# Retention, mixture of experts and MLP on one core: unstacked outputs, paced loads, shifted weight rounding

## The reference

```python
scores = scale * q @ k.T                  # batch 2, heads 8, sequence 576, head size 64
ret = scores * Dmat                       # gamma_h ** (i - j) for i >= j, else 0
x = ret @ v                               # as 1152 tokens x 512
for e in range(4):                        # mixture of experts, F = 1024
    out += p[:, e] * (relu(x @ w1[e]) @ w2[e])
h = out @ w_in                            # MLP, 2048 wide
y = (h * tanh(softplus(h))) @ w_out
```

## Time and profile before

| | us |
|---|---|
| median of three runs (lowest, highest) | 621.39 (620.98, 622.14) |
| profiled execution: its own time | 619.39 |
| profiled execution: span | 617.3 |
| PE busy | 604.9 (98% of the span) |
| PE weight loads busy | 546.4 (89%) |
| DVE, ACT, POOL busy | 265.1, 234.8, 278.5 (43%, 38%, 45%) |
| mean granted TensorE clock, share of full | 0.997 |
| DMA, mean | 82 GB/s |

### The profile page before, as it was taken

How to read it: one execution, slowest core, us unless ns; L and a number is a source line. 1 busy time by engine, 2 the same in 40 slices (tenths; PEclk the granted TensorE clock), 3 DMA queues, 4 the chain that set the end, 5 groups by cost and what they waited for, 6 DMA issues and landing times.

```text
span 617.3 us, 9709 instructions
## 1 busy us (share of the span) xinstructions
PE 604.9 (98%) x3952; PEld 546.4 (89%) x3952; DVE 265.1 (43%) x365; ACT 234.8 (38%) x434; POOL 278.5 (45%) x230
## 2 busy tenths in 40 slices
PE   7799999999999999999999999999999999999997
PEld 5788999999899999999999999989989999989996
DVE  5477654323254433154434154535545432334334
ACT  2466244322233321323332223435455454334431
POOL 2668645534435535335554435532446543443300
PEclk9899999999999999999999999999999999999999
DMA  9963222322112332012331112321112232201002
GB/s 345 340 225 103 72 66 65 109 72 64 35 34 69 107 100 69 34 35 69 102 102 54 50 35 69 103 68 52 52 35 65 67 101 75 69 0 52 2 0 103
DMA packets 24923, 50.47 MB, mean 82 GB/s; under 512 B 2864, under 2 KB 2992, under 8 KB 24880
## 3 DMA queue, kind: packets, MB, share of 16 engines
q1 hardware_dynamic: 24736, 49.84, 25.2%
q10 hardware_dynamic: 144, 0.02, 0.0%
HBM read 47.49 MB, written 2.36 MB: 81 GB/s over the span
## 4 chain that ended last, share of the span: by engine, by line
PE 95%; DMA 2%; issue 1%; DVE 1%; SPq 1%; ACT 1%
PE bank L527 31%; PE bank L529 31%; PE bank L528 31%; DMA w_raw<-in_weights 2%; PE bank L651 1%; PE bank L459 1%; PE bank L489 1%; PE bank L493 1%; SPq L423 0%; DVE acc_sb L945 0%; DVE acc_sb L949 0%; PE bank L464 0%; SPq L420 0%; ACT st L728 0%; ACT xa_hi L734 0%
## 5 line engine op out<-in xcount | busy, mean ns | idle before, releaser
L412 POOL TENSOR_TENSOR w_lo<-w_raw,w_hi 128x512 fp32r<-128x512 f32 x96 | 134.4, 1414 | 147.8 <-ACT w_hi L385 144.3
L527 PE MATMUL bank<-w_hi,h_hi 128*128 128x512 f32 x432 | 168.7, 390 | 0.0
L529 PE MATMUL bank<-w_hi,h_lo 128*128 128x512 f32 x432 | 168.4, 390 | 0.0
L528 PE MATMUL bank<-w_lo,h_hi 128*128 128x512 f32 x432 | 168.3, 390 | 0.0
L932 DVE TENSOR_TENSOR h_act<-part,bank 128x384 f32<-128x384 f32 x96 | 52.9, 552 | 170.4 <-PE bank L529 169.9
L407 POOL TENSOR_TENSOR ws<-ws_f,ws 128x1024 fp32r<-128x1024 f32 x24 | 58.4, 2432 | 144.8 <-ACT ws L381 144.8
L529 PEld LDWEIGHTS bank<-w_hi,h_lo 128*128 128x128 f32 x432 | 81.1, 188 | 16.9
L528 PEld LDWEIGHTS bank<-w_lo,h_hi 128*128 128x128 f32 x432 | 81.1, 188 | 12.3
L527 PEld LDWEIGHTS bank<-w_hi,h_hi 128*128 128x128 f32 x432 | 81.0, 188 | 12.1
L764 ACT ACTIVATE part<-bank 128x384 f32<-128x384 f32 x72 | 35.4, 491 | 138.8 <-PE bank L529 138.8
L899 DVE SCALAR_TENSOR_TENSOR h_lo<-h_act,h_hi 128x384 fp32r<-128x384 f32 x64 | 73.3, 1155 | 20.9 <-ACT h_hi L754 20.3
(11 more groups left out here) (98 smaller groups left out, 867.6 us busy)
## 6 DMA issues: line engine op xcount, KB each, us to landing
w_raw<-in_weights SPq DMA_DIRECT2D x144, 256.0 KB, 2.7
loaded<-in_toks SPq DMA_DIRECT2D x9, 512.0 KB, 7.7
loaded<-in_feats SPq DMA_DIRECT2D x8, 512.0 KB, 7.0
out<-acc_sb SPq DMA_DIRECT2D x6, 256.0 KB, 2.1
out<-acc_sb SPq DMA_DIRECT2D x1, 768.0 KB, 3.5
loaded<-in_first SPq DMA_DIRECT2D x1, 726.0 KB, 4.5
ident<-in_ident SPq DMA_DIRECT2D x1, 64.0 KB, 4.7
p_nat<-in_probs ACTq DMA_DIRECT2D x1, 18.0 KB, 5.3
```

The lines of the kernel that those rows point to most:

```text
L412: pool.tensor_tensor(w_lo[layer][:, x], w_raw[:, r % RAW], w_hi[layer][:, x].bitcast(F32), ALU.subtract).then_inc(s_wl, 1)
L527: pe.matmul(out, w[0], x[0], start=first, stop=False, **more)
L528: pe.matmul(out, w[0], x[1], start=False, stop=False, **more)
L529: return pe.matmul(out, w[1], x[0], start=False, stop=last, **more)
```

## The change

- The stacked chunks go: every chunk has its features in the usual halves, and `output` is `of_state` and `of_chunk` for chunks 1 and 2 too. `v_decay_again` goes, POOL decays both halves of the values, and DVE masks in one instruction.
- SP's loads are paced from chunk 4 on by waits for earlier ones to land: first two, then three are under way at a time. One weight block is loaded per chunk instead of two, and the next ones go out with three under way up to the fourteenth. `ident` is loaded before the fifteenth.
- The rounding jobs move about a turn later, ("s", 0, 0) from turn 7 to turn 9, behind ("w2", 0, 3) to ("w2", 0, 5) instead of ahead of them. ACT's part of it moves behind `t_hi` n = 1, ahead of the jobs of stage 1. In turn 3 ACT does one job ahead of tile 0. POOL does the jobs of a turn ahead of its `v_decay`.

```diff
-STACKED = 1, 2
-JOBS_IN = {1: (("w1", 0, 0),), 2: (("w1", 0, 1), ("w1", 0, 2)), 3: (("w1", 0, 3),), 4: (("w1", 0, 4), ("w1", 0, 5)),
-           5: (("w1", 0, 6),), 6: (("w1", 0, 7), ("w2", 0, 0)), 7: (("w2", 0, 1), ("w2", 0, 2), ("s", 0, 0)),
-           8: (("w2", 0, 3), ("w2", 0, 4)), 9: (("w2", 0, 5),)}
-WEIGHTS_IN = (2, 2, 2, 2, 2)
+JOBS_IN = {2: (("w1", 0, 0),), 3: (("w1", 0, 1), ("w1", 0, 2)), 4: (("w1", 0, 3),), 5: (("w1", 0, 4),),
+           6: (("w1", 0, 5), ("w1", 0, 6)), 7: (("w1", 0, 7), ("w2", 0, 0)), 8: (("w2", 0, 1), ("w2", 0, 2)),
+           9: (("w2", 0, 3), ("w2", 0, 4), ("w2", 0, 5), ("s", 0, 0))}
+PACED = 14
@@ SP @@
-            at = 0
-            for c in range(SLOTS, PLACES):
-                for r in range(at, at + WEIGHTS_IN[c - SLOTS]):
-                    load_weights(r)
-                at += WEIGHTS_IN[c - SLOTS]
+            load_weights(0)
+            feats_there(SLOTS - 1)
+            sp.wait_ge(s_o, 1)
+            load_feats(SLOTS)
+            weights_there(0)
+            load_toks(SLOTS)
+            feats_there(SLOTS)
+            load_weights(1)
+            toks_there(SLOTS)
+            for c in range(SLOTS + 1, PLACES):
+                at = c - SLOTS + 1
+                feats_there(c - 1)
                 sp.wait_ge(s_o, c - SLOTS + 1)
                 load_feats(c)
+                toks_there(c - 1)
+                if c == SLOTS + 1:
+                    weights_there(1)
                 load_toks(c)
-            sp.dma_start(ident[:, :], ident_in).then_inc(s_id, 16)
-            for r in range(at, len(LOADS)):
+                weights_there(at - 1)
+                load_weights(at)
+            for r in range(PLACES - SLOTS + 1, len(LOADS)):
+                if r < PACED:
+                    weights_there(r - 3)
+                if r == PACED:
+                    sp.dma_start(ident[:, :], ident_in).then_inc(s_id, 16)
                 load_weights(r)
@@ PE @@
-                if c in STACKED:
-                    pe.wait_ge(s_va, c)
...
-                if c in STACKED:
-                    pe.wait_ge(s_xt, c)
-                    pe.wait_ge(s_st, 2 * c)
-                    pe.wait_ge(s_sm, c + 1)
-                    for hp in range(PAIRS):
-                        for b in range(BATCH):
-                            of_both(c, b, 2 * hp)
-                            mm = of_both(c, b, 2 * hp + 1)
-                    mm.then_inc(s_o, 1)
-                    return
@@ ACT @@
+                ahead = 1 if c in TILE_AMID else 0
+                for job in IN_TURN.get(c, ())[:ahead]:
+                    job_hi(act, job)
                 if c in TILE_AMID:
                     plain_hi(*divmod(TILE_AMID[c], ITEMS))
-                for job in IN_TURN.get(c, ()):
+                for job in IN_TURN.get(c, ())[ahead:]:
                     if JOBS[job][0] != "s":
                         job_hi(act, job)
             for n in range(4):
                 t_hi(0, n)
                 if n == 1:
+                    for job in IN_TURN[PLACES]:
+                        if JOBS[job][0] == "s":
+                            job_hi(act, job)
                     for job in IN_STAGE[1]:
                         job_hi(act, job)
@@ DVE @@
-                if c in STACKED:
-                    for b in range(BATCH):
-                        op = dve.tensor_tensor(masked_scores(c, b), ps_s[c % SCORES][HALF[b]],
-                                               mask[HALF[b]].unsqueeze(1).broadcast_to([CH, HEADS, CH]), ALU.mult)
-                    op.then_inc(s_sm, 1)
-                    return
...
-                    v_decay_again(1)
...
-                    v_decay_again(2)
@@ POOL @@
             for c in range(TURNS):
+                for job in IN_TURN.get(c, ()):
+                    job_lo(pool, job)
                 if c + 2 < PLACES:
                     v_decay(c + 2)
-                for job in IN_TURN.get(c, ()):
-                    job_lo(pool, job)
```

More of the change, by code:

```diff
@@ L252, in build @@
         s_vd = sem("s_vd")
-        s_va = sem("s_va")
         s_sc = sem("s_sc")
@@ L285, in build, with k_feats, q_feats, v_toks @@
         s_out = sem("s_out")
[L287 to L312, removed]
+        def k_feats(c):
+            return slots[:, c % SLOTS, 0]
+        def q_feats(c):
+            return slots[:, c % SLOTS, 1]
+        def v_toks(c):
+            return slots[:, c % SLOTS, 2]
+        def k_toks(c):
+            return slots[:, c % SLOTS, 3]
+        def masked_scores(c):
+            return k_feats(c)
         def landed(c):
@@ L430, in load_weights, with feats_there, toks_there, weights_there @@
                   .then_inc(s_raw[r % RAW], 16)
+            def feats_there(c):
+                sp.wait_ge(s_feats[c % SLOTS], landed(c))
+            def toks_there(c):
+                sp.wait_ge(s_toks[c % SLOTS], landed(c))
+            def weights_there(r):
+                sp.wait_ge(s_raw[r % RAW], 16 * (r // RAW + 1))
             sp.dma_start(loaded[:, lead - CONSTS:lead + 2 * KIND], first_in).then_inc(s_feats[0], 16)
@@ L458, in score @@
             def score(c, b, h):
-                return pe.matmul(ps_s[c % SCORES][HALF[b], h], k_feats(c, b)[:, h], q_feats(c, b)[:, h],
+                return pe.matmul(ps_s[c % SCORES][HALF[b], h], k_feats(c)[HALF[b], h], q_feats(c)[HALF[b], h],
                                  start=True, stop=True)
             def state(c, b, h):
-                return pe.matmul(ps_state[HALF[1 - b], h], k_toks(c, b)[:, h], v_toks(c, b)[:, h],
+                return pe.matmul(ps_state[HALF[1 - b], h], k_toks(c)[HALF[b], h], v_toks(c)[HALF[b], h],
                                  start=c == 0 and h == 0, stop=True, skip_group_check=True)
@@ L488, in of_state @@
             def of_state(c, b, h):
[L489 removed]
+                return pe.matmul(ps_o[HALF[h % 2], b, h // 2], st[HALF[b], (c - 1) % 2, h], q_feats(c)[HALF[b], h],
                                  start=h < 2, stop=False, skip_group_check=True)
             def of_chunk(c, b, h):
[L493 removed]
+                return pe.matmul(ps_o[HALF[h % 2], b, h // 2], v_toks(c)[HALF[b], h], masked_scores(c)[HALF[b], h],
                                  start=c == 0 and h < 2, stop=True, skip_group_check=True)
[L496 to L498 removed]
             def output(c):
                 pe.wait_ge(s_vd, c + 1)
[L503 to L512 removed]
                 if c > 0:
@@ L723, in state_copy @@
                     act.wait_ge(s_o, c)
-                if c + 1 in STACKED:
-                    act.wait_ge(s_va, c + 1)
                 for b in range(BATCH):
-                    to = state_and_v(c + 1, b)[HALF[1 - b]] if c + 1 in STACKED else st[HALF[b], c % 2]
-                    act.activation(to, ps_state[HALF[1 - b]], ACT.Copy).then_inc(s_st, 1)
+                    act.activation(st[HALF[b], c % 2], ps_state[HALF[1 - b]], ACT.Copy).then_inc(s_st, 1)
             def first_hi(c):
@@ L856, in masked @@
                 dve.wait_ge(s_sc, c + 1)
-                if c in STACKED:
-                    for b in range(BATCH):
-                        op = dve.tensor_tensor(masked_scores(c, b), ps_s[c % SCORES][HALF[b]],
-                                               mask[HALF[b]].unsqueeze(1).broadcast_to([CH, HEADS, CH]), ALU.mult)
-                    op.then_inc(s_sm, 1)
-                    return
-                dve.tensor_tensor(slots[:, c % SLOTS, 0], ps_s[c % SCORES],
-                                  mask.unsqueeze(1).broadcast_to([P, HEADS, CH]), ALU.mult).then_inc(s_sm, 1)
-            def v_decay_again(c):
-                dve.wait_ge(s_toks[c % SLOTS], landed(c))
-                by = key_decay[HALF[1], c].unsqueeze(2).broadcast_to([CH, HEADS, DH])
-                dve.tensor_tensor(v_toks(c, 1), slots[HALF[1], c % SLOTS, 2], by, ALU.mult).then_inc(s_va, 1)
+                dve.tensor_tensor(masked_scores(c), ps_s[c % SCORES], mask.unsqueeze(1).broadcast_to([P, HEADS, CH]),
+                                  ALU.mult).then_inc(s_sm, 1)
             def rows(i):
@@ L1002, in _ @@
                     decayed(c - 1)
-                if c == 1:
-                    v_decay_again(2)
                 if c > PER_BLOCK + 1:
@@ L1091, in v_decay @@
                 pool.wait_ge(s_toks[c % SLOTS], landed(c))
-                rows = HALF[0] if c in STACKED else slice(0, P)
-                v = slots[rows, c % SLOTS, 2]
-                by = key_decay[rows, c].unsqueeze(2).broadcast_to([rows.stop, HEADS, DH])
-                pool.tensor_tensor(v, v, by, ALU.mult).then_inc(s_vd, 1)
+                pool.tensor_tensor(v_toks(c), v_toks(c), key_decay[:, c].unsqueeze(2).broadcast_to([P, HEADS, DH]),
+                                   ALU.mult).then_inc(s_vd, 1)
             pool.wait_ge(s_feats[0], landed(0))
@@ L1143 @@
     weights = [halves(moe_w1[e], moe_w2[e]) for e in range(MOE_EXPERTS)] + [halves(moe2_w_in, moe2_w_out)]
-    feats = np.stack([by_features(k), by_features(q)], axis=3)
-    for c in STACKED:
```

(3 more changed lines are left out.)

1 line of the change is left out of this document (removed).

## The result

The changed kernel took 624.84 us, the median of six runs (624.37 to 630.69), beside 621.56 for the kernel before (six runs, 620.84 to 623.09): 1.0073 times as long, 95% interval 1.0051 to 1.0095. In a later session on another chip it took 623.85 (twelve runs) beside 620.53, 1.0063 (1.0039 to 1.0087); one of the twelve, 630.97, lies over 1.5% above the fastest and is left out of the ratio. The ratios here are worked out from the single runs; the medians divided give 1.0053 in both sessions. By the medians the kernel is slower by 3.3 us, where 0.5 us less was forecast.

What follows compares the result with a forecast made beforehand. PE was taken as busy without a gap from 50 us on, idling 8.9 us before, mostly for instructions. Front - 2.4 and stage 2 + 1.9 made - 0.5 us against the median 621.39: 620.9 us, range 617.8 to 624.2.

Steps and rivals of the forecast that it cites:

- stage 2: Rounding jobs on POOL and ACT up to P6: moved later, they make PE idle 1.9 us (1.0 to 2.8) there.
- the four additions: POOL's last job, the sum, ahead of P6: 0.75 us each undisturbed, 0.9 beside busy DVE, ending at 64.1 to 64.7.
- The front: From the start to the end of tile 6: ends at 48.7 us against 51.05, 2.4 us gained.
- The bound and the stalls: PE idles 8.9 us before 50 us, none after; it runs out of instructions at about every 254th.
- ACT's queue behind the additions: Rounding, two weights, two `t_hi` and `keep` ahead of P6: 4.4 us, so bank 6 is empty at 68.5.
- The rival that P6 would not wait: At P6, POOL or DVE is quicker together than thought, so only the front counts: 619.0 us, chance 0.15.
- rival 5: Ahead of P6, PE's idle time lets the clock fall, up to 1.6 us more: 622.5 us, chance 0.07.
- the turnaround: Length of a stretch of 254 PE instructions in the front: 4.4 us, at a DMA share of some 0.7.
- The wait ahead of tile 0: In the front, PE waits for chunk 2's split: 1.2 us idle, hidden before by the 2.3 us stall.
- The first stall's end: PE's first wait for instructions in the front: its end goes from 14.73 to 14.2 us.
- The unstacked passes: Scores and state of turns 0 and 1: each loses about 0.9 us, most of the 1.8 turning into waiting.
- rival 6: Whole kernel: pacing changes no stall, passes give 1.7 us, stage 2 takes 1.9: 621.6 us, chance 0.05.

Runs made afterwards that it cites:

- pad114: The kernel before with its 7 start warm-up matmuls of 512 columns replaced by 64 of 56, 114 more instructions: 621.82 us beside 621.26, ratio 1.0007.
- fill_p6: The changed kernel with 16 matmuls of zeros on an unused bank right ahead of P6: 622.90 us beside 620.70 for the kernel before, ratio 1.0046.
- s_early: The changed kernel with job ("s", 0, 0) moved back from turn 9 to turn 7: 622.92 us beside 620.79 for the kernel before, ratio 1.0039.
- jobs_only: The kernel before with only the rounding jobs moved, stacked chunks and unpaced loads kept: 625.80 us beside 620.79, ratio 1.0096.
- after_again: The changed kernel run once more, in a later session on another chip: 623.85 us beside 620.53 for the kernel before, ratio 1.0063.
- unpaced: The changed kernel with the kernel before's load order, without pacing: 625.93 us beside 620.79 for the kernel before, ratio 1.0099.
- after_ahead: The changed kernel with ACT's roundings put ahead of its waits for tiles: 620.23 us beside 620.53 for the kernel before, ratio 0.9990.
- stacked_after: The changed kernel with stacked chunks 1 and 2 put back, pacing and moved jobs kept: 623.33 us beside 620.70 for the kernel before, ratio 1.0044.

## Why the prediction was wrong

Against the forecast of 620.9 us the kernel took 624.84, 3.9 more. Two steps of stage 2 failed and account for most of it: the four additions were priced too low (P6 1.5 us later than forecast), and the clock's fall at P6 was priced at nothing (1.6 us or more). The front gave 0.4 to 1.0 us less than forecast.

- **The bound and the stalls** were read rightly. PE's idle time lies in the front, the issue stalls come every 253 instructions (`pad114`), and what is lost later is lost in full.
- **Stage 2** was the right mechanism at the wrong size. The forecast had `keep` done at 68.5 by way of ACT's queue behind the additions, and P6 1.9 us late; it is done at 70.1, and P6 3.45 us late. The term that was mis-sized is the four additions: 3.0 to 3.6 us forecast, 5.2 measured. They start where I had them (60.9), and ACT's queue behind them is 3.9 us, not 4.4. The prediction took 0.75 us for one, from additions beside which DVE was idle or read PSUM, and 0.9 beside a busy DVE, for which it shows no row. They took 0.92 to 1.47, beside DVE instructions whose two inputs both lie in SBUF. The rival that P6 would not wait fell.
- **The clock** was rival 5, with a chance of 0.07 and 1.6 us. It fell in all five profiles with the 3 us wait (among them the change's two). In two it fell 0.8 us behind P6's start, for 3.4 us, and cost 1.6; in three it fell 0.6 to 1.0 us ahead of P6's start, for 6.8 us, and cost 2.8 to 2.9. `fill_p6` takes it away. This follows in part from the first error: behind the 1.96 us wait of `s_early`, about what I had forecast for P6, and behind 1.34 us the clock stayed. But behind a stall of 2.3 us it had fallen, and the range of the forecast wait went up to 2.8 us, so a chance of 0.07 was too small.
- **The front** was forecast 2.4 us better. By the medians, the change against `jobs_only`, it is 1.4 to 2.0 better; 54.42 against 54.34 in the profiles compares an execution with a late clock to one with an early one. The step that failed is the turnaround. I took 4.4 us for seven stretches, worked out from a DMA share of 0.7. The first took 3.97 and 5.07 us in the change's two profiles, the later ones 5.2 at 0.85, and the length does not follow the share. The loads that are held back lie under the later stretches. That the total came near is in part luck: the forecast end of tile 6 was 48.7 us, and `after_again` has it at 51.0. The wait ahead of tile 0, forecast at 1.2 us, was 2.2 there and 0.6 to 1.4 in other profiles with this front.
- **The first stall's end** was forecast at 14.2, from a profile whose clock was early. Where it was early it ended at 14.3 to 14.5 (`unpaced`, `s_early`, `after_ahead`); where it was late, near 16.0.
- **The unstacked passes** took 1.1 us instead of 2.0, as forecast, and the gain turned into waiting, as forecast. The part alone costs 1.4 to 1.8 us, which the forecast did not have; whether the clock has a share in that is not shown.
- **The sum**: - 2.4 + 1.9 + 0 was forecast; about - 1.7 for the front, + 3.4 for the wait and + 1.6 for the clock were measured, + 3.3. The first of these is a difference of medians from two sessions, the others are from profiles, so the agreement is no closer than 1 us. What the Trainium skill states in "Runtime: NRT & Kernel Launch", section "Instruction fetch mechanics" (rival 6), that the fetch of instructions is mostly hidden, does not hold for such small matmuls: `pad114` shows PE stalling by the count of them.

## What to carry to other kernels

A job queue moved back as a whole is late with its last member: follow every queue (here POOL's and ACT's in-order roundings) to its end, and price each entry at what it takes beside the very instructions that will then run on the other engine, not beside "a busy engine". Where a wait of some us opens on PE, count the clock's fall behind it as part of the wait's price. And before an engine's jobs are moved to later turns, see whether it can do them ahead of a wait it has anyway; here that was worth about 4 us. Compare the start of two profiles before comparing their fronts: here it moved the first stall by some 1.6 us.

## What the runs showed of the hardware

- PE can stall for its instructions at every 252nd to 254th matmul or weight load when these are small (`pad114`). From one stall's end to the next it took 3.8 to 6.9 us for the first such stretch, and the DMA share beside it did not decide how long: 3.97 us at 0.69, 5.02 at 0.76 and 5.07 at 0.57 with the same front, 4.87 at 1.01 and 6.38 at 1.03 in two unpaced ones.
- The 16 KB transfer of the next instructions began 1.6 to 4.4 us behind a stall's end, took 1.0 to 1.3 us, and PE resumed 1.2 to 1.6 us after it, where it waited for it.
- Pacing the loads gave 1.6 to 3.2 us by the ratios. In single profiles the issue waits of the front sum to 7.6 us in `unpaced` and to 4.7 and 7.4 in the changed kernel, 4.7 in `jobs_only` and 3.0 in `stacked_after`.
- POOL's 128x256 additions take 0.73 to 0.76 us alone and beside DVE instructions that read a PSUM bank, and 0.9 to 1.5 beside DVE instructions with both inputs in SBUF.
- Waits of 3.0 us on PE, five of five, went with half the clock for 3.4 or 6.8 us; two of 1.34 us and one of 1.96 did not.
- The clock reached full speed 4.4 to 5.3 us after the start in five of the profiles and 8.9 to 10.7 us after it in the nine others, though the start of all but `pad114` is the same code. In the unstacked kernels the first stall ends at 14.3 to 14.5 us in the first case and near 16.0 in the second.

What stays open: why the price of unstacking is, by the ratios, 1.2 to 1.8 us in three pairs and within the noise in the two others, how much of it is the clock, and what holds an instruction transfer back for 1.7 us in one execution and 2.9 in another of the changed kernel.
